# A top-1 expert layer's routing: the index of the fixed tiles is made from the rank alone, everything else about the places behind it

## The reference

```python
# 1: attention, 4 batches x 8 heads x 576 positions x 64, two kinds of sparse mask
x = attention(q, k, v)                       # -> (2304, 512)
# 2: skip or one of eight experts per row
do_compute = x @ w_skip > 0
logits = x @ w_gate                          # (2304, 8)
e_idx  = argmax(logits, axis=1)
gate_w = softmax(logits)[e_idx]
x[do_compute] += gate_w * (relu(x @ w1[e_idx]) @ w2[e_idx])   # 512 -> 1024 -> 512
# 3: MLP on all rows
h = x @ w_in                                 # 512 -> 2048
out = maximum(0.01 * h, h) @ w_out           # 2048 -> 512
```

## Time and profile before

| | |
|---|---|
| time, median of 3 runs | 775.92 us (771.88 to 779.18) |
| the profiled execution | 777.4 us |
| its span, first to last instruction | 775.2 us |
| TensorE busy | 716.9 us, 92% of the span |
| VectorE, ScalarE, GpSimd busy | 36%, 34%, 23% |
| mean granted TensorE clock | 0.974 of full |

### The profile page before, as it was taken

One profiled execution on the slowest core, in us unless ns is written; L12 is line 12 of the kernel. 1 busy time (PEld: TensorE's weight loads), 2 busy tenths in 40 slices (PEclk: granted clock), 3 DMA queues, 4 the chain that ended last, 5 costly groups with the idle time before them and its releaser, 6 DMA issues.

```text
span 775.2 us, 12846 instructions
## 1 busy us (share of the span) xinstructions
PE 716.9 (92%) x4628; PEld 664.1 (86%) x4628; DVE 276.2 (36%) x578; ACT 262.0 (34%) x522; POOL 180.5 (23%) x182
## 2 busy tenths in 40 slices
PE   2989979993699999998999999999999999999997
PEld 2878868873699999997999999998989899999986
DVE  4667656757100000003332333233333333332222
ACT  4687666651111112212222223322232322222222
POOL 2120100011686666562100310040031004001000
PEclk9999998986699999999999999999999999999999
DMA  8483746779799999972100210030012004001001
GB/s 175 107 188 100 168 102 171 218 236 229 168 317 341 300 314 338 315 248 64 43 1 0 70 54 1 7 116 1 1 59 63 0 0 122 0 0 41 1 0 41
DMA packets 73112, 91.46 MB, mean 118 GB/s; under 512 B 26704, under 2 KB 47728, under 8 KB 73073
## 3 DMA queue, kind: packets, MB, share of 16 engines
q1 hardware_dynamic: 63969, 66.14, 29.7%
q0 software_dynamic: 8048, 24.79, 11.3%
q10 hardware_dynamic: 1056, 0.02, 0.1%
HBM read 73.91 MB, written 17.01 MB: 117 GB/s over the span
## 4 chain that ended last, share of the span: by engine, by line
PE 74%; SPq 10%; DMA 5%; DVE 3%; issue 3%; ACT 2%; another core or an unknown queue 2%; ACTq 0%; DVEq 0%; POOLq 0%
PE psum L1584 26%; PE psum L1603 26%; PE psum L1497 8%; PE psum L1513 8%; SPq L401 6%; DMA x_rows<-xo 3%; SPq L396 2%; SPq L386 1%; ACT kt L797 1%; PE psum L1336 1%; PE psum L1523 1%; PE psum L1566 1%; DMA x_sb<-x_rows 1%; SPq L409 1%
## 5 line engine op out<-in xcount | busy, mean ns | idle before, releaser
L1584 PE MATMUL psum<-x2h,wih 128*128 128x384 f32 x384 | 130.6, 340 | 1.9 <-DVE x2l L1256 1.9
L1274 DVE SCALAR_TENSOR_TENSOR g_act<-g_raw 128x384 f32<-128x384 f32 x96 | 53.6, 558 | 219.4 <-ACT g_raw L960 205.9
L1584 PE MATMUL psum<-x2h,wil 128*128 128x384 f32 x384 | 129.5, 337 | 0.0
L1584 PE MATMUL psum<-x2l,wih 128*128 128x384 f32 x384 | 129.0, 336 | 0.0
L960 ACT ACTIVATE g_raw<-psum 128x384 f32<-128x384 f32 x96 | 47.2, 492 | 235.3 <-PE psum L1584 232.0
L1603 PE MATMUL psum<-woh,g_l 128*128 128x512 f32 x288 | 114.0, 396 | 0.0
L1603 PE MATMUL psum<-wol,g_h 128*128 128x512 f32 x288 | 113.7, 395 | 0.0
L1603 PE MATMUL psum<-woh,g_h 128*128 128x512 f32 x288 | 112.1, 389 | 0.7 <-DVE g_l L1278 0.7
L1497 PE MATMUL psum<-xt,wring 128*128 128x160 f32 x512 | 80.9, 305 | 0.6 <-issue 0.6
L759 POOL DMA_INDIRECT out_dram<-o_sb,idxo x15 | 15.9, 1061 | 277.8 <-ACT o_sb L955 274.8
L1513 PE MATMUL psum<-hp,wring 128*128 128x160 f32 x512 | 77.6, 299 | 0.0
(11 more groups left out here) (177 smaller groups left out, 899.2 us busy)
## 6 DMA issues: line engine op xcount, KB each, us to landing
wring<-in_moe_w_dram SPq DMA_DIRECT2D x64, 512.0 KB, 8.6
y_rows<-zrow SPq DMA_DIRECT2D x1, 4800.0 KB
q_st<-in_q_dram SPq DMA_DIRECT2D x8, 576.0 KB
k_st<-in_k_dram SPq DMA_DIRECT2D x8, 576.0 KB
x_sb<-x_rows SPq DMA_DIRECT2D x4, 1024.0 KB, 6.4
stage<-in_moe_w_in_dram POOLq DMA_DIRECT2D x4, 1024.0 KB, 9.0
stage<-in_moe_w_out_dram POOLq DMA_DIRECT2D x4, 1024.0 KB, 9.2
vs<-in_v_dram SPq DMA_DIRECT2D x20, 128.0 KB, 7.6
```

Of the source, the lines that this page charges most:

```text
L1274: dve.scalar_tensor_tensor(out=g_act[:, f % 2, :], in0=g_raw[:, f % 2, :], scalar=LEAK, in1=g_raw[:, f % 2, :], op0=ALU.mult, op1=ALU.max) ...
L1584: last = pe.matmul(bank[f % 2][:, 0:MT * P], wt[:, c, f * P:(f + 1) * P], xp[:, T.par, c, :], start=(c == 0 and n == 0), stop=(c == KD - 1 ...
```

## The change

The index of the eight fixed tiles (sixteen halves, HB) no longer waits for slots. For a token of expert e and rank r < 160 the half is 2e, plus 1 if r is 80 or more, and the row is r or r - 80; h80, r80, far and hid0, row0 give this, and far or a constant of 1000 puts skipped and overflowing tokens outside the columns. The remaining 28 halves (HO) get an index of their own, from slots, inside tile 0. In detail:

- comb, a stack of two 9x9 identities, takes the place of the 18x18 identity in the product that makes LOG, so that it adds the two parts. The copy and the addition on VectorE are gone.
- The one-hot takes fewer steps: eqp from sh, and kskip in place of the product with takes.
- Behind the rank: h80, far, r80, hid0, row0, comparisons over 16 halves (eq_b, all 18 tiles in one) and 80 rows (row_b, two parts), products on ScalarE and VectorE (none on GpSimd), 18 matmuls of 32 columns, tok_idx for the sixteen halves.
- Overflow counts and plan follow; then slots, rows, eq_o and row_o, their products (all on VectorE), record slots, gates, and the records' places (s_rec).
- TensorE makes TIDX_O, 18 matmuls of 56 columns, in tile 0 behind share(6); VectorE turns it into the rest of tok_idx.
- Both halves of the first x copy are on ScalarE.
- GpSimd: iteration 0 only gathers; scatters, weight loads and splits are one iteration later each, iteration 1 first waits for the overflow index, and the last iteration holds two splits.

The core of the diff:

```diff
@@ gpsimd: behind the first gather @@
             for i in range(2 * NU):
                 pool.wait_ge(s_xt, 2 * (i + 1))
                 gather_x(i + 1)
-                if i < 6:
+                if i == 0:
+                    continue
+                if i == 1:
+                    pool.wait_ge(s_tok_o, 1)
+                if i < 7:
                     pool.wait_ge(s_rec, 1)
                     carry()
-                    sort_rows(NT // 6 * i, NT // 6 * (i + 1))
-                if i == 6:
+                    sort_rows(NT // 6 * (i - 1), NT // 6 * i)
+                if i == 7:
                     pool.wait_ge(s_sct, 16 * NT)
                     pool.dma_start(srt[:, :, :], rec_d.rearrange("(t p) w -> p t w", p=P)
                                    ).then_inc(s_srt, 16)
-                if i + 1 < 2 * NU:
-                    if i:
-                        pool.wait_ge(s_stl, i)
-                    stage_load(i + 1)
-                stage_split(i)
+                if i > 1:
+                    pool.wait_ge(s_stl, i - 1)
+                stage_load(i)
+                stage_split(i - 1)
+            stage_split(2 * NU - 1)
@@ scalar @@
+            act.wait_ge(s_eqb, 1)
+            act.activation(tok_b[:, :, 0, :], eq_b[:, :, :], ACT.Copy, scale=c_p[:, 0:1]).then_inc(s_hot, 1)
             x_copy(0, 0)
+            act.wait_ge(s_xt, 2)
+            act.activation(xt[:, 0, :, HALF:TILE],
+                           bank[3][:, 0:KD * HALF].rearrange("d (c t) -> d c t", c=KD),
+                           ACT.Copy).then_inc(s_xf[1], 1)
@@ vector: from the logits @@
-            step(dve.tensor_copy(ls[:, :, :], LOG[:, :, 0:E + 1]))
-            step(dve.tensor_tensor(ls[:, :, :], LOG[:, :, E + 1:LW], ls[:, :, :], ALU.add))
+            skips = LOG[:, :, E]
+            step(dve.reduce_max(lmax[:, :], LOG[:, :, 0:E], AX.X))
+            dve.tensor_tensor(sh[:, :, :], LOG[:, :, 0:E], free(lmax[:, :], T3, 2), ALU.subtract
+                              ).then_inc(s_sh, 1)
+            dve.wait_ge(s_sh, 1)
+            step(dve.scalar_tensor_tensor(out=eqp[:, :, :], in0=sh[:, :, :], scalar=0.0,
+                                          in1=free(c_pref[:, :], T3, 1), op0=ALU.is_ge, op1=ALU.mult))
+            dve.tensor_scalar(ohb[:, 0:NT, 0], skips, 0.0, None, ALU.is_le).then_inc(s_one, 1)
+            step(dve.reduce_max(kmax[:, :], eqp[:, :, :], AX.X))
+            step(dve.scalar_tensor_tensor(out=kskip[:, :], in0=skips, scalar=0.0, in1=kmax[:, :],
+                                          op0=ALU.is_le, op1=ALU.add))
+            dve.tensor_tensor(ohb[:, 0:NT, 1:E + 1], eqp[:, :, :], free(kskip[:, :], T3, 2), ALU.is_equal
+                              ).then_inc(s_one, 1)
@@ vector: behind the rank @@
+            step(dve.tensor_tensor(posn[:, :, :], RANK[:, 0:NT, :], ohb[:, 0:NT, 1:E + 1], ALU.mult))
+            step(dve.reduce_sum(rank[:, :], posn[:, :, :], AX.X))
+            dve.scalar_tensor_tensor(out=h80[:, :], in0=rank[:, :], scalar=float(HALF), in1=half2[:, :],
+                                     op0=ALU.is_ge, op1=ALU.add).then_inc(s_r, 1)
+            dve.tensor_scalar(far[:, :], rank[:, :], float(TILE), 1000.0, ALU.is_ge, ALU.mult
+                              ).then_inc(s_r, 1)
+            dve.tensor_scalar(r80[:, :], rank[:, :], float(HALF), -float(HALF), ALU.is_ge, ALU.mult
+                              ).then_inc(s_r, 1)
+            n_[0] += 3
+            dve.wait_ge(s_r, n_[0])
+            dve.tensor_tensor(hid0[:, :], h80[:, :], far[:, :], ALU.add).then_inc(s_r, 1)
+            n_[0] += 1
+            step(dve.tensor_tensor(row0[:, :], rank[:, :], r80[:, :], ALU.add))
+            HB3, R3 = [P, NT, HB], [P, NR, HALF]
+            dve.tensor_tensor(eq_b[:, :, :], free(hid0[:, :], HB3, 2), free(c_half[:, 0:HB], HB3, 1),
+                              ALU.is_equal).then_inc(s_eqb, 1)
+            dve.tensor_tensor(row_b[:, 0:NR, :], free(row0[:, 0:NR], R3, 2), free(c_row[:, :], R3, 1),
+                              ALU.is_equal).then_inc(s_rowb, 1)
+            dve.wait_ge(s_eqb, 1)
+            dve.tensor_tensor(tok_b[:, :, 1, :], eq_b[:, :, :], free(c_t[:, :], HB3, 2), ALU.mult
+                              ).then_inc(s_tokt, 1)
+            dve.tensor_tensor(row_b[:, NR:NT, :], free(row0[:, NR:NT], R3, 2), free(c_row[:, :], R3, 1),
+                              ALU.is_equal).then_inc(s_rowb, 1)
...
+            dve.wait_ge(s_ti, 1)
+            step(dve.tensor_copy(tok_t[:, 0:HB], TIDX[:, 0:HB]))
+            dve.scalar_tensor_tensor(out=tok_idx[:, 0:HB], in0=TIDX[:, HB:2 * HB], scalar=float(P),
+                                     in1=tok_t[:, 0:HB], op0=ALU.mult, op1=ALU.add).then_inc(s_plan, 1)
@@ tensor @@
-                        last = pe.transpose(LOG[:, 2 * j + u, :], lt[:, j % 2, u * P:(u + 1) * P],
-                                            ident[0:LW, 0:LW])
+                        last = pe.matmul(LOG[:, 2 * j + u, :], lt[:, j % 2, u * P:(u + 1) * P],
+                                         comb[:, :], start=True, stop=True)
...
+                last = pe.matmul(TIDX, row_b[:, t, :], tok_b[:, t, :, :].rearrange("p a h -> p (a h)"),
+                                 start=(t == 0), stop=(t == NT - 1))
...
+                    if first and f == 8:
+                        for hf in range(2):
+                            pe.wait_ge(s_xf[hf], 2)
+                        pe.wait_ge(s_hot_o, 3)
+                        for t in range(NT):
+                            last = pe.matmul(TIDX_O, row_o[:, t, :],
+                                             tok_o[:, t, :, :].rearrange("p a h -> p (a h)"),
+                                             start=(t == 0), stop=(t == NT - 1))
+                        last.then_inc(s_ti_o, 1)
```

More of the change, by code:

```diff
@@ L132, in attention_experts_mlp @@
     lt = at(r, "lt", [2 * (E + 1), 2, 2 * P])
-    ls = at(r, "ls", [P, NT, E + 1])
     lmax = at(r, "lmax", [P, NT])
+    eqp = at(r, "eqp", [P, NT, E])
+    kskip = at(r, "kskip", [P, NT])
+    selp = at(r, "selp", [P, NT, E + 1])
+    half2 = at(r, "half2", [P, NT])
+    rank = at(r, "rank", [P, NT])
+    h80 = at(r, "h80", [P, NT])
+    r80 = at(r, "r80", [P, NT])
+    far = at(r, "far", [P, NT])
+    hid0 = at(r, "hid0", [P, NT])
+    row0 = at(r, "row0", [P, NT])
     sh = at(r, "sh", [P, NT, E])
     ex = at(r, "ex", [P, NT, E])
-    eq = at(r, "eq", [P, NT, E])
     kmax = at(r, "kmax", [P, NT])
-    oh = at(r, "oh", [P, NT, E])
     notk = at(r, "notk", [P, NT])
@@ L155, in attention_experts_mlp @@
     row = at(r, "row", [P, NT])
-    eq_half = at(r, "eq_half", [P, NT, NHALF])
-    oh_tok = at(r, "oh_tok", [P, NT, 2, NHALF], BF16)
-    oh_row = at(r, "oh_row", [P, NT, HALF], BF16)
+    HB, HO = 2 * E, NHALF - 2 * E
+    eq_b = at(r, "eq_b", [P, NT, HB], BF16)
+    eq_o = at(r, "eq_o", [P, NT, HO], BF16)
+    tok_b = at(r, "tok_b", [P, NT, 2, HB], BF16)
+    tok_o = at(r, "tok_o", [P, NT, 2, HO], BF16)
+    row_b = at(r, "row_b", [P, NT, HALF], BF16)
+    row_o = at(r, "row_o", [P, NT, HALF], BF16)
     tok_t = at(r, "tok_t", [HALF, NHALF])
@@ L602, in _ @@
                                     base=0, pattern=[[1, P]], channel_multiplier=-1))
+            step(pool.tensor_tensor(comb[:, :], ident[0:LW, 0:E + 1], ident[0:LW, E + 1:LW], ALU.add))
+            assert count[0] == POOL_COMB
             def carry():
@@ L647, in _ @@
             step(pool.iota(pos_i[:, HEAD:NT], pattern=[[P, MT]], base=P * HEAD, channel_multiplier=1))
+            step(pool.memset(c_e2[:, 0:1], 1000.0))
             assert count[0] == POOL_ALL
[L650 to L655, removed]
             def gather_x(j):
@@ L1113, in _ @@
-            step(dve.tensor_tensor(ohb[:, 0:NT, 1:E + 1], oh[:, :, :], free(takes[:, :], T3, 2), ALU.mult))
-            assert n_[0] == R_ONEHOT
+            skips = LOG[:, :, E]
[5 more added lines that the diff above has]
+                                          in1=free(c_pref[:, :], T3, 1), op0=ALU.is_ge, op1=ALU.mult))
@@ L1116, in _ @@
+            C9 = [P, NT, E + 1]
+            step(dve.tensor_tensor(selp[:, :, :], ohb[:, 0:NT, :], free(c_e2[:, :], C9, 1), ALU.mult))
+            step(dve.reduce_sum(half2[:, :], selp[:, :, :], AX.X))
+            step(dve.tensor_scalar(takes[:, :], skips, 0.0, None, ALU.is_gt))
             step(dve.tensor_scalar(notk[:, :], takes[:, :], -float(SKIP), float(SKIP),
                                    ALU.mult, ALU.add))
-            dve.wait_ge(s_rex, 1)
-            step(dve.reduce_sum(esum[:, :], ex[:, :, :], AX.X))
@@ L1181, in _ @@
-            dve.tensor_copy(plan[:, :], planf[:, :]).then_inc(s_plan, 1)
+            HO3, RO3 = [P, NT, HO], [P, NT, HALF]
+            step(dve.tensor_tensor(eq_o[:, :, :], free(hidx[:, :], HO3, 2), free(c_half[:, HB:NHALF], HO3, 1),
+                                   ALU.is_equal))
+            dve.tensor_tensor(row_o[:, :, :], free(row[:, :], RO3, 2), free(c_row[:, :], RO3, 1),
```

(13 more changed lines are left out.)

114 lines of the change are left out of this document (45 added, 69 removed).

## The result

| | before | after |
|---|---|---|
| time, median of 20 runs each | 773.29 us | 778.8 us |
| ratio, 95% interval | | 1.0067 (1.0054 to 1.008) |
| profiled execution's span | 775.2 us | 776.7 us |
| mean granted clock | 0.974 | 0.972 |

The change makes the kernel 5.2 us slower (0.67%, 4.2 to 6.2), where 2.2 us less had been forecast. The two spans differ by 1.5 us alone, because in the profile of after the attention stage happened to end earlier: its last logits leave TensorE at 175.15, against 178.97 before. Counted from there, after is 1.5 + 3.8 = 5.3 us longer, which agrees with the measurement.

What follows compares the result with a forecast made beforehand. TensorE was taken as the bound from the first expert tile on, so an earlier index moves everything behind it. Index -5.1, overflow matmuls +1.0 and GpSimd's tail +1.9 gave -2.2 us from 775.92: 773.7 us, range 769.5 to 779.5.

Steps and rivals of the forecast that it cites:

- Logits, +0.3: Logit transposes replaced by float32 products with comb: three pairs on the chain, 0 to +0.6 us, taken as +0.3.
- Before and behind the rank: VectorE's routing steps either side of the rank matmuls: savings of 1.16 us before and 4.28 us behind.
- Index to first tile ... this stays: From written index to first expert matmul, 8.47 us: plan words hidden behind the gather, first 24 matmuls' 5.38 us unchanged.
- the sign of being wrong: First gather: the prediction called itself wrong if this took 10 us, where about 5.3 us was expected again.
- Rival C: First gather queues behind the zero fill, so the 5.1 us are lost: +2.9 us, 778.8 us; chance 0.15.
- E: Rival in tile 0: VectorE's list outlasts the cover of s_rec, 2 us late costs 2 us, 775.7 us; chance 0.10.
- Overflow index, +1.0: Tile 0: eighteen more matmuls of 56 columns in TensorE's queue, between 0.5 and 1.7 us, taken as +1.0.
- GpSimd's tail: Last iteration: two splits end 10.5 us later, last y gather lands 2.8 us late, MLP starts +1.9 us, up to +3.4.
- B: Rival at the MLP's start: the tail is hidden and TensorE doesn't wait, -4.1 us, 771.8 us; chance 0.15.
- D: Rival: two more idle us make the clock fall at the MLP's start, costing 2.2 us, 775.9 us; chance 0.15.

Runs made afterwards that it cites:

- a_tail_swap2: a_tail_swap with SyncE queueing expert 0's last four weight pieces only when the first half of the gathered rows has been transposed; ratio 0.9929 to before.
- b_swap2: The kernel before with the same order of SyncE's queue as a_tail_swap2, nothing else; ratio 0.999.
- a_tail_late: a_tail with the zero fill of y_rows issued by ScalarE behind its first x copies, SyncE waiting for it before tile 7; ratio 1.0061 to before.
- the six kernels of the table: after, a_warm, a_dvewait, a_tail, b_tail and before: same fill and weight loads, index at different times; first expert matmul 34.5 to 35.7 us behind the fill's issue.
- a_warm: The changed kernel with 38 spare transposes on TensorE where it waits for the MLP's first rows; ratio 1.0043 to before.
- a_dvewait: The changed kernel with VectorE's list behind the plan waiting until the first gathered rows have landed and been transposed; a single run, 780.45 us.
- b_tail: The kernel before with only GpSimd's loop of the change, without a wait for an overflow index; ratio 1.0058.
- b_swap: The kernel before with the zero fill queued ahead of the last four weight pieces of expert 0 on SyncE; ratio 1.0023.
- a_tail: The changed kernel with GpSimd's work caught up in early iterations, so that only one split stands in the last; ratio 0.9984 to before.
- a_tail_swap: a_tail with SyncE queueing the zero fill ahead of the last four weight pieces of expert 0; ratio 0.9966 to before.
- a_tail_pieces: a_tail with the zero fill cut in six 800 KB pieces behind SyncE's weight loads in tiles 1 to 6; ratio 1.0012 to before.
- _early: The two kernels a_early and b_early, with ratios 1.0117 and 1.013 to before.
- _late: a_tail_late, ratio 1.0061, and the kernel before with the same late zero fill, nothing else, ratio 1.0089.
- _pieces: a_tail_pieces, 1.0012, and the same six fill pieces on the kernel before, 1.004, and on the changed kernel with its own GpSimd loop, 1.004.
- a_early: The changed kernel with the zero fill issued by GpSimd in three parts during attention instead of by SyncE; ratio 1.0117 to before.
- b_early: The kernel before with the same early zero fill as a_early; ratio 1.013.

## Why the prediction was wrong, point by point

- **Logits, +0.3: too small.** The products' four records for a pair of tiles take 0.54 us for the 0.22 of two transposes (two records of 0.135 a product, for one of 0.11), so three pairs on the chain cost about 1.0.
- **Before and behind the rank: right.** The one-hot was complete 1.98 us behind lmax's start (175.24 to 177.22), predicted 1.97; from there to the index 6.95 (to 184.17), against 1.7 + 5.36 = 7.06. The index is 14.6 - 9.0 = 5.6 us nearer to the logits' end, for 1.16 + 4.28 = 5.44 predicted; with the logits' own 1.0 the gain is 4.6, for 5.1. a_tail_swap2 beside b_swap2 (4.7 us) shows that this can be had.
- **"Index to first tile ... this stays": the step that failed.** The 8.47 us were taken as a property of the gather. 5.33 of them were the gather's first half beside the end of the fill. Alone, TensorE can start on the first half 3.2 to 3.3 us behind its issue, and the second has landed 4.4 to 4.5 behind that issue (b_swap2: 192.20 to 196.61; a_tail_late: 185.98 to 190.46). Started with 8.8 us of the fill to run, the first half alone took 10.55, over the 10 us that the prediction itself had named as the sign of being wrong. Rival C had this, with its condition and its sign, and the argument against it was wrong: 5.33 is indeed not much above the 3.9 of an unloaded y gather, but only because little of the fill was left at that start; it said nothing about an earlier one. The Trainium skill (DMA: Bandwidth & Descriptors, Queues, rings and completion order) says that an engine takes packets from its queues in turn, and the sum was weighed by that. The trace doesn't bear out a small transfer slipping through: 10.55 us beside the fill for 3.2 without it. Whether the order is a strict one it doesn't settle: in the six kernels of the table the first half never landed ahead of the fill's end, but its distance behind it was 0.5 to 1.8 us, and not fixed.
- **E: wrong.** VectorE's list ended with pos_i at 195.71 + 0.17; share(0) came at 202.95 and waited for nothing. It wasn't the late gather that saved this: in a_tail_swap2 the list ended at 195.51, and share(0) came at 196.20 without a wait.
- **Overflow index, +1.0: about right.** L1596 took 0.84 us in TensorE's timeline. The tiles as a whole took no longer, as a stall of 0.69 us that before had at tile 1 is not there in after.
- **GpSimd's tail: mechanism right, size off.** The last y gather is issued 2.01 us behind the last yt copy, where before it was 9.44 ahead: 11.45 later, for 10.5 predicted. And it takes longer: 5.11 us for the gather on the chain, where 3.9 had been taken from the earlier trace rows. All three y tiles were late. The chain runs through the second of them and then through the last eight transposes, which took 2.04 us at the lower clock, where 0.5 had been estimated for four:

```profile
351.21 5.11 DMA y<-y_rows,idx
...
356.42 0.76 DVE y L1298
357.18 0.04 issue
357.23 2.04 PE psum L1624 x8
```

+4.6 in all for +1.9 predicted, above the prediction's own upper end of +3.4. B is refuted with it.
- **D: came as well.** The 2.2 us that it named were 2.0 in the profile and 1.9 in a_warm's time. But its condition isn't settled: the clock fell with the long wait in after, a_dvewait and b_tail, yet also in b_swap, b_swap2 and a_tail_swap2, with 5.66, 5.48 and 5.46 us from the last yt copy to the MLP, and not in before, a_tail and a_tail_swap, with 5.56, 5.73 and 5.64. A stretch of a_tail_swap2, whose first 24 MLP matmuls took 6.0 us for the 4.4 of a_tail:

```profile
352.00:354.00 2.00, 2.00 (x8) 2.00 (x8) 0.00 (x0) 0.00 (x0) 1.01 (x1) 0.50 0.00 0
```

- **The choice of cases.** C, D and the tail's size were priced alone, as alternatives. They have separate causes and came together: -1.0 in place of -4.1 up to the last yt copy, +4.6 and +2.0 in place of +1.9 behind it. C and D together would have given +2.9 + 2.2 = +5.1 us, for the 5.2 of the ratio. (The median of 778.8 is C's figure by coincidence: before's own median in those runs was 2.6 us under the one that the prediction started from.)

**Open.** Why bulk bytes hold a gather so long isn't shown, only that they do and how much. What ScalarE waited for in the tiles of a_tail_late and a_tail_pieces isn't either. What lets the clock fall at the MLP's start in some kernels with a short wait isn't either; part of the difference between any two of these kernels may come from it. That a_tail is 6.4 us under after, where the tail alone cost before 4.5 (b_tail), lies within their intervals.

## What to carry to other kernels

A transfer's time beside others is not a price for it at another start: before an index is made earlier, ask what is still queued in the DMA engines at the new start, and move those bytes too. Work that is pushed one iteration later costs nothing until the last iteration; count there what two steps take together with their landings, and add the clock to any wait that TensorE gets. Cases with separate causes are priced together as well as alone.

## What the runs showed of the hardware

- An indirect gather of 2 x 80 rows of 2 KB, with nothing large beside it: TensorE could start on the first half 3.2 to 3.3 us behind the first issue, and both had landed at 4.3 to 4.7 us (the _early, _late and _pieces kernels and b_swap2). Beside the 4.8 MB of writes from another queue the first half took 6.6 to 10.6 us when 6 to 9 us of them were left to run, and 5.3 us with 4 left. Beside 2 MB of weight reads as the last bytes queued ahead it took 6.7 and 8.3 us (b_swap, a_tail_swap). In the second gather one half took up to 12.1 us.
- The place of the same 4.8 MB of zeros, with GpSimd caught up: ratio 0.9984 beside the first gather (a_tail), 1.0061 beside the second (a_tail_late), 1.0012 in pieces in the tiles (a_tail_pieces, where 4.5 of 5.9 us stand beside waits that the profile doesn't name), and 0.9929 directly behind the x tiles with the weights held back (a_tail_swap2). In attention they cost more than any of these, 1.0117 (a_early) and 1.013 (b_early).
- Where TensorE had spare transposes in its wait the granted clock stayed at 1.00; in after it fell to 0.50, and the 2 us from 354 in which it fell had TensorE busy for 0.47. That alone doesn't decide it: in a_tail_swap the clock stayed at 1.00 in and behind a stretch with TensorE busy 0.28 of 2 us:

```profile
354.00:356.00 2.00, 0.28 (x3) 0.04 (x1) 1.75 (x3) 1.19 (x3) 0.00 (x0) 1.00 0.59 164
```

- One issue of an indirect gather on GpSimd took 2.38 us (a_dvewait) and one 1.50 us (a_early) beside VectorE's row_o and tok_o, for 1.0 to 1.2 us otherwise.
